# GpSimd adds the key squares in front of the norms' products, with the expert weights' jobs spread over groups 4 to 11, in an attention and mixture-of-experts kernel

## The reference

```python
# u, v: (8, 3072, 256)   z: (8, 3072, 64)
scores = matmul(z, z.T) / 3072
attn = maximum(scores, 0.0) ** 2
x = (u * matmul(attn, v)).reshape(8 * 3072, 256)

logits = x @ w_gate                       # 8 experts
expert = argmax(logits, axis=1)
gate_w = softmax(logits)[expert]
# expert e takes its first 768 tokens in order, the rest are dropped
h = maximum(disp[e] @ w1[e], 0.0)         # w1: (8, 256, 1024)
y = h @ w2[e]                             # w2: (8, 1024, 256)
out[token] = gate_w * y                   # 0 for dropped tokens
```

## Time and profile before

| | |
|---|---|
| median of 3 runs | 869.6 us |
| the profiled execution | 869.84 us |
| span of its core, first to last instruction | 868.1 us |
| around the span | 1.7 us |
| mean granted TensorE clock | 0.999 |
| TensorE busy | 854.4 us, 98% |
| VectorE busy | 632.7 us, 73% |
| ScalarE busy | 574.6 us, 66% |
| GpSimd busy | 121.5 us, 14% |

### The profile page before, as it was taken

The page is one execution under the profiler, slowest core; times in us unless marked ns, Lnnn a source line. Parts: engine busy times, 40 slices in busy tenths (PEclk is TensorE's granted clock), DMA queues, the critical chain, the costliest instruction groups (busy, mean ns, idle before and its releaser), DMA issues.

```text
span 868.1 us, 22767 instructions
## 1 busy us (share of the span) xinstructions
PE 854.4 (98%) x7257; PEld 684.0 (79%) x7258; DVE 632.7 (73%) x1380; ACT 574.6 (66%) x874; POOL 121.5 (14%) x121
## 2 busy tenths in 40 slices
PE   6999999999999999999999999999999999999997
PEld 5888888888888887888888888888677777777776
DVE  7976877988888988788888798687465655565531
ACT  6978786868778679787778777678344434435422
POOL 0001101101101110110110110110112121211212
PEclk9999999999999999999999999999999999999999
DMA  7923254354323662432442441721725325315101
GB/s 288 352 74 112 68 164 155 83 167 136 106 75 115 232 165 76 139 93 63 134 108 55 127 134 44 273 72 36 129 83 171 84 92 163 136 52 151 55 18 36
DMA packets 127797, 104.52 MB, mean 120 GB/s; under 512 B 90669, under 2 KB 115322, under 8 KB 126752
## 3 DMA queue, kind: packets, MB, share of 16 engines
q1 hardware_dynamic: 122880, 91.61, 35.7%
q0 software_dynamic: 4896, 12.64, 4.1%
HBM read 40.03 MB, written 44.93 MB: 98 GB/s over the span
## 4 chain that ended last, share of the span: by engine, by line
PE 93%; DVE 2%; issue 2%; ACT 1%; DMA 1%; SPq 1%; ACTq 0%; POOL 0%; DVEq 0%; POOLq 0%
PE O L664 16%; PE O L668 16%; PE O L666 16%; PE Sc L775 14%; PE Sc L629 8%; PE Sc L630 8%; PE O L798 3%; PE O L800 3%; PE O L802 3%; PE M L798 2%; PE M L800 2%; PE M L802 2%; PE M L705 1%; ACT Sc L451 0%; DMA x<-disp 0%
## 5 line engine op out<-in xcount | busy, mean ns | idle before, releaser
L664 PE MATMUL O<-vS,attn_hi 128*128 128x256 f16 x1332 | 363.0, 273 | 1.3 <-DVE vS L917 1.2
L668 PE MATMUL O<-vS,attn_lo 128*128 128x256 f16 x1332 | 363.0, 273 | 0.0
L666 PE MATMUL O<-vS,attn_hi 128*128 128x256 f16 x1332 | 363.0, 273 | 0.0
L451 ACT ACTIVATE Sc<-Sc 128x768 f32<-128x768 f32 x224 | 178.0, 795 | 87.8 <-PE Sc L630 79.0
L934 DVE TENSOR_TENSOR attn_lo<-attn,attn_hi 128x768 f16<-128x768 f32 x223 | 213.7, 958 | 7.7
L455 ACT ACTIVATE attn<-Sc 128x768 f32<-128x768 f32 x224 | 181.8, 811 | 7.1
L664 PEld LDWEIGHTS O<-vS,attn_hi 128*128 128x128 f16 x1332 | 130.3, 98 | 28.8 <-issue 1.4
L666 PEld LDWEIGHTS O<-vS,attn_hi 128*128 128x128 f16 x1332 | 130.3, 98 | 26.4
L629 PE MATMUL Sc<-zP 128*128 (+1 forms) x450 | 146.5, 326 | 1.6 <-DVE zP L900 0.9
L630 PE MATMUL Sc<-zQ,zP 128*128 (+1 forms) x450 | 146.4, 326 | 0.0
L928 DVE CAST attn_hi<-attn 128x768 f16<-128x768 f32 x223 | 123.7, 555 | 30.2 <-ACT attn L455 26.2
(11 more groups left out here) (155 smaller groups left out, 911.6 us busy)
## 6 DMA issues: line engine op xcount, KB each, us to landing
out<-empty SPq DMA_DIRECT2D x16, 1536.0 KB, 6.4
wraw<-in_moe_w SPq DMA_DIRECT2D x16, 1024.0 KB
rawv<-in_v SPq DMA_DIRECT2D x14, 768.0 KB, 7.7
ubuf<-in_u SPq DMA_DIRECT2D x19, 384.0 KB, 3.2
disp<-vS SPq DMA_DIRECT2D x8, 774.0 KB, 8.8
rawz<-in_z SPq DMA_DIRECT2D x3, 768.0 KB
xT<-xrow SPq DMA_TRANSPOSE x54, 2.4
disp<-xrow,slot POOLq DMA_INDIRECT x54
```

Source lines behind the costliest of these rows:

```text
L451: act.activation(pair, pair, ACT.Relu).then_inc(s["relu_done"], 1)
L664: nc.tensor.matmul(o_part(t), hi, v[:, 0:D], start=c == 0 and j == 0 and t % 2 == 0, stop=False, skip_group_check=True)
L666: nc.tensor.matmul(o_part(t), hi, v[:, D:2 * D], start=False, stop=False, skip_group_check=True)
L668: ins = nc.tensor.matmul(o_part(t), lo, v[:, 0:D], start=False, stop=c == PAIRS - 1 and j == 1, skip_group_check=True)
```

## The change

Five edits:

1. `fold`: in group 2 of a batch, behind this group's scatter, GpSimd waits for the squares of `zsq` and adds the right half to the left, and then the second quarter to the first. The norms of the next group multiply only this quarter, by four products of 96 columns each where there were four of 384. The norms at the start are as they were.
2. The weights' jobs get new positions, one to a double for an engine: `w_max` of expert 0 at double 6 of groups 4, 5, 6, 7 (in the branch for g > 3), of expert 1 at (8, 8), (9, 9), (10, 9), (11, 6); `all_w` at n = 7 and n = 12; `w_scales` (8, 6); high parts (8, 7), (8, 8), (8, 10), (9, 10); low parts (9, 6), (9, 7), (10, 6), (10, 7).
3. At the start the memsets of `onesb` and `ones` stand ahead of 25 small memsets.
4. `first_z(2)` runs the sum L946 between its low part and its copies; it stood behind them.
5. SyncE's wait for the load of `u` moves behind the transpose of `x0` and `zero_out`, for groups from 1 on.

```diff
@@ SyncE, body
-                wait_apart(sp, s["loaded_u"], n * 16 + 16)
-                if not isinstance(n, int):
+                if isinstance(n, int):
+                    sp.wait_ge(s["loaded_u"], 16)
+                else:
                     wait_apart(sp, s["due_ready"], n * 2)
...
                     only_if(sp, n <= ZERO_PIECES, zero_out)
+                    wait_apart(sp, s["loaded_u"], n * 16 + 16)
                     wait_apart(sp, s["loaded_early"], n * 16)
@@ GpSimd, body
+                def fold():
+                    wait_apart(pool, s["norm_step"], (n & 120) + 8)
+                    pool.tensor_tensor(zsq[:, 0:2 * GROUP], zsq[:, 0:2 * GROUP], zsq[:, 2 * GROUP:4 * GROUP], ALU.add
+                                       ).then_inc(s["fold_step"], 8)
+                    wait_apart(pool, s["fold_step"], (n & 120) * 2 + 8)
+                    pool.tensor_tensor(zsq[:, 0:GROUP], zsq[:, 0:GROUP], zsq[:, GROUP:2 * GROUP], ALU.add
+                                       ).then_inc(s["fold_step"], 8)
                 def rest():
+                    only_if(pool, g == 2, fold)
                     only_if(pool, g == 3, reduce_maxes)
-                    only_if(pool, n == 8, lambda: all_w(0))
-                    only_if(pool, n == 9, lambda: all_w(1))
+                    only_if(pool, n == 7, lambda: all_w(0))
+                    only_if(pool, n == 12, lambda: all_w(1))
@@ TensorE, group 3, double 6
-                                wait_apart(pe, s["norm_step"], (n & 120) + 8)
-                                norms().then_inc(s["nrm_psum"], 8)
+                                wait_apart(pe, s["fold_step"], (n & 120) * 2 + 16)
+                                for k in range(4):
+                                    part = slice(k * (GROUP // 4), (k + 1) * (GROUP // 4))
+                                    ins = nc.tensor.matmul(M[0][:, part], onesb[:, :], zsq[:, part], start=True, stop=True,
+                                                           skip_group_check=True)
+                                ins.then_inc(s["nrm_psum"], 8)
@@ VectorE, start
+            dve.memset(onesb[:, :], 1.0)
+            dve.memset(ones[:, :], 1.0).then_inc(consts, 1)
             for e in range(E):
                 dve.memset(rank[:, :, e:e + 1], float(E - e))
...
-            dve.memset(onesb[:, :], 1.0)
-            dve.memset(ones[:, :], 1.0).then_inc(consts, 1)
@@ VectorE, first_z
                 z_lo(to, h, col)
+                if between is not None:
+                    between()
                 dve.tensor_copy(hi_across[out, to:to + SLICE * P], hi[own, to:to + SLICE * P]).then_inc(s["khi_ready"], 2)
@@ VectorE, body
-                            only_if(dve, g < 4, lambda: first_groups(c))
+                            with dve.If(g < 4):
+                                first_groups(c)
+                            if c == W_MAX0_AT:
+                                with dve.Else():
+                                    for q in range(4):
+                                        only_if(dve, n == 4 + q, lambda: w_max(0, 0, q))
@@ constants
-W_MAX_AT = (6, 7, 8, 9)
-W_SCALES_AT = 10
-W_HI_IN = ((9, 9), (9, 10), (11, 6), (11, 7))
-W_LO_IN = ((10, 6), (10, 7), (11, 9), (11, 10))
+W_MAX0_AT = 6
+W_MAX1_IN = ((8, 8), (9, 9), (10, 9), (11, 6))
+W_HI_IN = ((8, 7), (8, 8), (8, 10), (9, 10))
+W_LO_IN = ((9, 6), (9, 7), (10, 6), (10, 7))
```

More of the change, by code:

```diff
@@ L196, in relu2_attention_moe @@
             h_ready hh_done hl_done y_summed y_ready y_scattered0 y_scattered1 y_scattered2
-            y_scattered3 fac_ready h_first hh_first due_ready loaded_early"""
+            y_scattered3 fac_ready fold_step h_first hh_first due_ready loaded_early"""
         s = {n: sem(n) for n in names.split()}
@@ L901, in z_lo_across, with first_z @@
                                 (zP if h else zQ)[own, bass.ds(to, SLICE * P)]).then_inc(s["klo_ready"], 2)
-            def first_z(q):
+            def first_z(q, between=None):
                 h, to, col = q // 2, q * SLICE * P, q % 2 * SLICE * P
@@ L943, in _, with sum_v @@
             first_z(1)
-            first_z(2)
-            dve.wait_ge(s["vparts0"], len(V0_PIECES) - 1)
-            dve.tensor_reduce(mx[:, 1:2], vsum[:, 0:len(V0_PIECES) - 1], AX.X, ALU.add).then_inc(s["vsum0"], 1)
+            def sum_v():
+                dve.wait_ge(s["vparts0"], len(V0_PIECES) - 1)
+                dve.tensor_reduce(mx[:, 1:2], vsum[:, 0:len(V0_PIECES) - 1], AX.X, ALU.add).then_inc(s["vsum0"], 1)
+            first_z(2, sum_v)
             dve.wait_ge(s["amx0"], 1)
@@ L1140, in first_groups @@
                 def first_groups(c):
-                    if c in (FCUR_AT, W_SCALES_AT, *W_MAX_AT):
+                    if c == FCUR_AT:
                         def group0():
[L1144 to L1152, removed]
+                            dve.tensor_copy(fcur[:, :], fnext[:, :]).then_inc(s["fcur_ready"], 8)
+                            only_if(dve, n == 8, lambda: w_scales(0, 0))
                         only_if(dve, g == 0, group0)
-                    if c in W_MAX_AT:
-                        only_if(dve, n == 9, lambda: w_max(1, 1, W_MAX_AT.index(c)))
+                    for q, (group, at) in enumerate(W_MAX1_IN):
+                        if c == at:
+                            only_if(dve, n == group, lambda: w_max(1, 1, q))
                     for q, (group, at) in enumerate(W_LO_IN):
```

## The result

The changed kernel takes 875.2 us in the median of five runs (874.66 to 878.02) against 869.9 before: 1.0067 times the time, 95% interval 1.0056 to 1.0079. It is 5.3 us slower. I had predicted 866.5 us, with 3 in 100 for a slowdown. The span of the profiled execution grew from 868.1 to 873.4 us.

A forecast was written before the change was run, and what follows sets the result against it. TensorE, busy in 98% of the span, bounds the kernel; 0.85 (start) + 0.96 (norms) + 0.81 (weights' jobs) + 0.52 (end of attention) = 3.14 us saved gives 866.5 us, range 866.0 to 868.1.

The forecast's parts named there:

- The fold itself is costed at nothing: GpSimd's additions in group 2: hidden, adding no time unless they hold VectorE.
- 21 us for two additions: GpSimd's time in group 2 between squares ready at 113.65 us and norms products at 134.70.
- The four parts: Savings summed to 3.14 us: start 0.85, norms 0.96, weights' jobs 0.81, end of the attention 0.52.
- The fold's rival: GpSimd's additions hold VectorE at L973 in groups 2 and 10; TensorE stalls 2.2 us, time 868.7; chance 0.11.
- My bound of 3.1 us for the two additions: GpSimd's fold: cost of both additions with two sources and a destination priced as three streams; 1.0 us with one.
- The end of the attention: SyncE's earlier transpose of x0 lets L775 start at 612.02 instead of 612.54: 0.52 us, range 0.3 to 0.55.
- Norms: Four products of 96 columns take 0.17 us instead of 0.65, twice in the loop: 0.96 us saved, bounds 0.86 and 0.98.
- Weights' jobs: Three stalls at ends of groups 8, 9, 11 go: 0.81 us, range 0.3 to 0.9; groups 4 to 7 stay covered.
- The second rival: Stalls come back: VectorE 0.5 us later before L973 in groups 4 to 7, 0.81 lost; 867.3 to 867.9; chance 0.08.
- Start: Earlier memsets of ones (0.35) and earlier value-scale sum (0.50) bring the first `weigh` 0.85 us forward; bounds 0.48 and 0.90.
- a margin of 0.2 us: At the start: first square ends at 16.73, VectorE needs it at 16.94, so it just fits.
- Clock: TensorE's clock rises only after the first scores, some 10 us longer at the low level: 871.4 or more; chance 0.03.

The follow-up runs named there:

- fold_only: Kernel before with edit 1 alone (GpSimd's two additions and the four norms products of 96 columns): 876.54 us, 1.0081.
- rewarmed: Changed kernel plus one useless GpSimd reduction over partitions of a zero column, straight behind the two additions: 870.77 us, 1.0010 against the kernel before.
- fold_between: Changed kernel with the zeroing transfer last and GpSimd's fold between a one-column scratch addition and a zero-column reduction: 867.08 us, 0.9969 against the kernel before.
- sync_only: Kernel before with edit 5 alone (SyncE's wait for u behind the transpose of x0 and the zeroing of out): 872.0 us, 1.0026.

## Why the prediction was wrong

**The step that failed** is "The fold itself is costed at nothing", with its account of GpSimd: "21 us for two additions". I priced the additions and asked only who waits for them. I did not ask what the next operation of another kind on GpSimd pays. Going over to an addition or back costs 6.0 to 7.1 us each time in the changed kernel, at MODIFY_POOL_CONFIG (`fold_only`'s expectation says 6.8 to 7.1 and misses the 6.0 of group 11; over all kernels it is 5.5 to 7.8). The way there is covered; the way back stands ahead of the maxima's reduction, on which VectorE's scales hang, and `gate_x` behind them, and `weigh` behind that. It cost 4.26 us of stalls. `rewarmed` shows it by moving the switch alone: 4.4 us. The trace of before held a hint that I passed over: after its memsets at the start GpSimd ran only reductions and scatters, and MODIFY_POOL_CONFIG stands just once, at 2.2 us, between the last memset and the first reduction, where nobody waits. The Trainium skill, "GPSIMD Engine Reference", section "2.1 Instruction dispatch", states that the first call of a freshly loaded kernel on GpSimd pays about 6 us from MODIFY_POOL_CONFIG on with no visible instruction. The trace agrees, at 6.0 to 7.1 us, and shows more: the price comes again at each change of kind.

**The sum.** The four parts that I had added up to 3.14 us came to 2.83 (0.54, 0.96, 0.81 and 0.52), with 0.28 from short stalls that I hadn't counted. What I had at nothing cost 8.4: 4.26 and 1.68 at the fold, 2.5 at the register loads.

**The fold's rival** had nearly the right size of loss by contention, and the wrong place. I had put the additions at 113.65, on `gate_x`; they came 7 us later, on VectorE's work early in groups 3 and 11, where it has less room. The changed kernel's time line in group 11:

```profile
377.32 2.65 DVE L1047 SCALAR_TENSOR_TENSOR xrow<-ubuf,rscale,xrow 128x256 f16<-128x256 f32 x3
379.89 1.30 DVE L947 CAST attn_hi<-attn 128x768 f16<-128x768 f32 x1
```

The same three took 1.27 us in group 9 of the kernel before, a high part 0.55. So VectorE is held for 1.4 and 0.75 us. It cost 1.68 us in three stalls, where I had 2.2 in two for the rival. `fold_between` has the additions where the rival had them, and the loss is 0.4 us: they had the room that I denied them there. My bound of 3.1 us for the two additions was not far off: they took 2.5 us in `fold_only` and 3.8 at 120.0 in the changed kernel.

**The end of the attention.** The gain of 0.52 came to the hundredth: L792 follows at 617.91, and the wait is now for TensorE's own sequencer (the row L792 of the waits), as I had read from L766. What I left out is the other transfer in the diff's lines. I took the move for one of a wait; but the zeroing stands behind that wait, so it came earlier too, and met the register loads on which TensorE's sequencer hangs. In group 9 it was issued at 322.80 in the kernel before, 0.8 us behind the start of TensorE's load, and at 320.57 in `sync_only`, 1.4 us ahead of it; in the changed kernel, 1.7 us ahead. In `sync_only` it cost 2.7 us against the 0.57 gained. This is the second term that the prediction had at nothing.

**Norms.** Predicted 0.17 us for four products, measured 0.17, 43 ns each. The line through 128 and 384 columns held. The 81 ns for 128 columns of the Trainium skill, "TensorE: Matmul & The Clock Gate", section "Back-to-back issue gap", are not what the rows show: 56 ns for 128 columns, 43 ns for 96 here.

**Weights' jobs.** Right in all three stalls, and in the cover. In group 7 I had 1.92 us of idle time against 1.9 of work; 0.70 were left, so the fourth call costs 1.2 us and not 1.9: right in the outcome, with a term that was too large. The second rival did not occur.

**Start.** The mechanism was right, the size 0.54 to 0.73 instead of 0.85. L865 moved by 0.77 and the memsets gave 0.34. The first square, which I had named as late next, was later in both traces than in that of before (end 17.02 and 17.21 against 16.73). It hangs on loaded values, and its end goes from 16.73 to 17.52 over all traces of this case, with the trace of before the earliest of them: in `sync_only`, whose start is that of before, it is 17.46. I had counted on a margin of 0.2 us in a time that a transfer sets and that I had read from a single, lucky trace. GpSimd did work beside the copies, at 0.60 instead of 0.37 us.

**Clock.** No part: the granted clock is 1.0 in the profiled execution. The idle products go from 107 to 56 ns apart at 9.0 us, in the kernel before at 9.5: ahead of the first scores in both, so this rival did not occur either.

## What to carry to other kernels

Before you give GpSimd one operation of another kind, find the next operation of the old kind on it and see who waits for that; if it is on the path, pay the switch early with a useless operation, or put the work on an engine that needs no switch. When a wait moves in a queue, list the transfers that stand behind it as well as the one that you want earlier, and look for what else is happening at their new time, short register loads included. When a margin hangs on a transfer, read it from more than one trace. A shorter piece of work on TensorE is worth nothing ahead of a wait that it only reaches sooner: the norms' 0.96 us counted in full only when no stall stood behind them.

## What the runs showed of the hardware that I had not expected

GpSimd waits 5.5 to 7.8 us between MODIFY_POOL_CONFIG and the operation when the kind changes between addition and reduction over partitions (6.0 to 7.1 in the changed kernel), and about 0.1 us when it doesn't. Its addition of 768 bf16 columns takes 1.62 to 2.36 us, one of 384 takes 0.91 to 1.41. Beside it, VectorE operations take up to 2.4 times as long: a high part 1.08 to 1.30 instead of 0.55, one low part 2.27 instead of 0.96; `gate_x`, which reads its products from PSUM, kept its 0.75. VectorE does the same two additions in 0.55 and 0.36 us. Loading one word from SBUF into a sequencer's register takes 0.3 us, also with the DMA engines 97% busy on the weights' transfer, and 0.9 while the zeroing transfer runs.
